# One DVE assignment step per query tile, placed differently in the second head of the first pair

## Chip, cores and metric

The kernel runs on one core of a Trainium2 chip. The metric is the device time of one execution in microseconds, as the median of repeated runs. Engines are named as in the profile: PE is the matrix engine (PEld its weight loads), DVE the vector engine, ACT the scalar engine, POOL GpSimd, SP the engine that only issues DMAs here.

## What is computed

Three stages follow each other: a clustered attention, a mixture of experts that sends each token to one of eight experts, and a gated dense layer. Only the first is touched. Its core:

```python
q_assign = np.argmax(np.einsum('bhsd,hcd->bhsc', q_n, c_n), axis=-1)
k_assign = np.argmax(np.einsum('bhsd,hcd->bhsc', k_n, c_n), axis=-1)
mask = q_assign[:, :, :, None] == k_assign[:, :, None, :]
scores = scale * np.matmul(q, k.transpose(0, 1, 3, 2))
scores = np.where(mask, scores, -1000000000.0)
attn = softmax(scores)          # row maximum, exp, row sum
out = np.matmul(attn, v)
```

There are 2 x 8 = 16 heads of 768 tokens with 64 channels, and 16 cluster centroids for each of the 8 head numbers. Every query and key gets the number of its nearest centroid, and a query sees only keys with the same number.

## The kernel before

Heads are worked through in pairs: pair 0, a hardware loop over the pairs 1 to 6, and pair 7. In a pair, slot 0 is the first head and slot 1 the second. A head has six query tiles of 128 rows, `qt` 0 to 5. Tiles are numbered through as `n = 6 * head + qt`, so the second head of pair 0 has the tiles 6 to 11.

Each engine has an instruction stream of its own, written by hand in program order, and the streams meet only at semaphores. An engine executes its stream in that order. For one query tile `n` they do this:

- PE `head` (L1465): the scores of tile `n` into one of two PSUM buffers (`score_high` L1402 and `score` L1423, two matmuls each); then the six transposes of the probabilities of tile `n - 2` (`transpose_probs`, L1433, in two groups of three, each waiting for DVE to have emptied the previous tile's group, `s_pl`); then, for the head before, a half of the product with v in the tiles with `qt % 3` of 0 and 1 (`probs_v`, L1448 to L1451), or the six small matmuls that turn its result back in the tiles with `qt % 3` of 2 (`turn_back`, L1461).
- DVE `head` (L1100): the row maximum of tile `n` (`neg_max`, L1110); two subtractions that empty the transposed probabilities of tile `n - 2` (`pT_lo`, L1078); in `qt` 0 the row sums of the head before (L1086, L1088); in `qt` 2 and 5 the scaling of its result (`scale_x`, L1097), which waits for `turn_back`.
- ACT `head` (L836): copies of the transposed probabilities of tile `n - 2` (L829), then the exponential of tile `n` (L849); in `qt` 1 and 4 the copy `o_T` (L834) that `turn_back` needs.

Beside this, each pair prepares the assignment masks of the next pair. PE makes the similarities (L1361). DVE finds the assignment in five steps (`assign`, L1051), each of 128x384 elements and each waiting for the one before: step 0 is the maximum (L1055), step 1 compares with it (L1058), step 2 multiplies with the centroid numbers (L1062), step 3 is the minimum (L1065), step 4 writes `one_hot` (L1069) and sends `s_hot`. PE then transposes `one_hot` (`hot_transposes`, L1384, six matmuls), ACT writes the mask rows from that (`make_mask_rows`, L821), and SP sends them by DMA to the operands of the next pair's heads (L471).

In pair 0, PE's `hot_transposes` stands at the end of the third query tile of the second head, behind `turn_back` and ahead of the scores of the fourth tile:

```python
if more and slot == 1 and qt == (2 if first else 1):
    hot_transposes(pp + 1)          # begins with pe.wait_ge(s_hot, pp)
```

ACT's `make_mask_rows` stands in the fourth query tile of that head. DVE runs its steps at the end of a query tile, behind everything else of that tile:

```python
if before and qt % GT == 2:
    scale_x(g - 1, pp - 1 + slot, 1 - slot, qt // GT)
for step in steps.get((slot, qt), ()) if more else ():
    assign(pp + 1, step)
```

`steps` says which steps run in which (slot, query tile). Pair 0 has a table of its own, `first`; there the similarities are ready only in the fifth query tile of its first head, so step 0 runs in (0, 5).

Of the kernel before, what the change touches and what calls it, by code (L numbers as in the profile page):

```python
# [22 lines left out]
def attention_moe_gate(nc, qT, kT, v, cen, w_gate, w1, w2, w_a, w_b, w_out, out):  # L23
# [32 lines left out]
    with ExitStack() as ctx:  # L56
# [316 lines left out]
        def static(j):  # L373
            return isinstance(j, int)
# [637 lines left out]
        def _(dve):  # L1012
# [38 lines left out]
            def assign(pp, step):  # L1051
                s3 = sims.rearrange("p (t c) -> p t c", c=C)
                if step == 0:
                    dve.wait_ge(s_sims, pp + 1)
                    dve.tensor_reduce(sim_max[:, :], s3, AX_X, ALU.max).then_inc(s_smax, 1)  # L1055
                if step == 1:
                    dve.wait_ge(s_smax, pp)
                    dve.tensor_tensor(sim_is_max[:, :, :], s3, sim_max[:, :].unsqueeze(2).to_broadcast([P, 4 * QT, C]),  # L1058
                                      ALU.is_equal).then_inc(s_sism, 1)
                if step == 2:  # L1060
                    dve.wait_ge(s_sism, pp)
                    dve.tensor_tensor(sim_idx[:, :, :], sim_is_max[:, :, :], c_minus_ps, ALU.mult).then_inc(s_sidx, 1)  # L1062
                if step == 3:
                    dve.wait_ge(s_sidx, pp)
                    dve.tensor_reduce(first_idx[:, :], sim_idx[:, :, :], AX_X, ALU.min).then_inc(s_sfst, 1)  # L1065
                if step == 4:
                    dve.wait_ge(s_sfst, pp)
                    dve.wait_ge(s_hotT, pp)
                    dve.tensor_tensor(one_hot[:, 2:, 0:C], c_minus_ps,  # L1069
                                      first_idx[:, :].unsqueeze(2).to_broadcast([P, 4 * QT, C]),  # L1070
                                      ALU.is_equal).then_inc(s_hot, 1)

            def evacuate(n, qt, pT_ps=pT_ps):
                half, j = qt // GT, qt % GT
                for part in range(2):
                    dst = (slice(None), half, slice(part * GT, (part + 1) * GT), slice(j * P, (j + 1) * P))
                    dve.wait_ge(s_ph, 2 * n + part + 1)
                    dve.tensor_tensor(pT_lo[dst], pT_ps[part].rearrange("p (k q) -> p k q", q=P),  # L1078
                                      pT_hi[dst].bitcast(F32), ALU.subtract).then_inc(s_pl, 1)

            def row_norm(g, slot):
                dve.wait_ge(s_exp, QT * (g + 1))
                if not static(g) or g >= 1:
                    dve.wait_ge(s_rinv, g)
                    dve.wait_ge(s_x, 2 * g)
                dve.tensor_reduce(row_eps[:, :], row_sum[:, slot], AX_X, ALU.add).then_inc(s_reps, 1)  # L1086
                dve.wait_ge(s_reps, g + 1)
                dve.reciprocal(row_inv[:, :], row_eps[:, :]).then_inc(s_rinv, 1)  # L1088

            def scale_x(g, stored, slot, half):  # L1090
                dve.wait_ge(s_back, 2 * g + half + 1)
                dve.wait_ge(s_rinv, g + 1)
                if half == 0 and (not static(g) or g >= 2):
                    dve.wait_ge(s_rows[slot], stored * 16)
                    dve.wait_ge(s_logit, g - 1)
                tiles = slice(half * GT, (half + 1) * GT)
                dve.tensor_tensor(x_head[:, slot, tiles, :], x_ps, row_inv[:, tiles].unsqueeze(2).to_broadcast([P, GT, XW]),  # L1097
                                  ALU.mult).then_inc(s_x, 1)

            def head(pp, slot):  # L1100
                g = pp * 2 + slot
                more = not static(pp) or pp + 1 < PAIRS
                before = not static(g) or g >= 1
                first = static(pp) and pp == 0
                steps = {(0, 5): (0,), (1, 0): (1, 2), (1, 1): (3, 4)} if first else {
                    (0, 2): (0,), (0, 3): (1,), (0, 4): (2,), (0, 5): (3,), (1, 0): (4,)}
                for qt in range(QT):
                    n = g * QT + qt
                    dve.wait_ge(s_S, n + 1)
                    dve.tensor_reduce(neg_max[:, qt % 2:qt % 2 + 1], scores[qt % 2][:, 0:S], AX_X, ALU.max,  # L1110
                                      negate=True).then_inc(s_max, 1)
                    if before or qt >= 2:
                        evacuate(n - 2, (qt - 2) % QT)
                    if before and qt == 0:
                        row_norm(g - 1, 1 - slot)
# [4 lines that stand above are left out]
                    if static(pp) and pp == PAIRS - 1:  # L1120
                        early_routing(slot * QT + qt)
# [29 lines left out]
            def early_routing(at):  # L1151
                if at == 0:
                    dve.wait_ge(s_hotr, PAIRS)
                    link(dve.tensor_copy(early_e_minus, e_minus[:, 0, :]))
                if at == 1:
                    dve.wait_ge(s_logit, H)
                    choose(0, 0)
                if at == 3:
                    choose(0, 1)
                if at == 4:  # L1160
                    choose(0, 2)
                    link(dve.tensor_copy(l_max[:, batch[0]], early_max))
                if at == 6:
                    choose(0, 3)
                if at == 7:
                    choose(0, 4)

            def pair(pp):
                head(pp, 0)
                head(pp, 1)  # L1170
# [628 lines left out]
```

## Time and profile before

| | |
|---|---|
| median of 3 runs | 816.57 us (816.55 to 816.61) |
| the profiled execution's own time | 816.57 us |
| its span, first to last instruction | 814.8 us |
| PE busy | 806.8 us, 99% of the span |
| DVE, ACT, POOL busy | 456.0, 361.1, 365.0 us |
| granted TensorE clock | 1.000 |

A row of the timeline gives the start of a group of like instructions, its length, the engine, the line, the operation, output and input tiles with their shapes, and how many there are; behind them, in brackets, idle time before it and what ended it. Instructions of one engine overlap at their ends, so the step from one start to the next is shorter than the length of a row. The steps from start to start are what an engine's program costs.

### The profile page before, as it was taken

The page shows a single profiled execution, that of the slowest core. Times are in us where ns is not written, and L with a number is a line of the kernel's source. Part 1 is how long each engine was busy: PE and PEld are TensorE (multiplying, and loading weights), DVE is VectorE, ACT ScalarE, POOL GpSimd, SP SyncE. Part 2 cuts the span into 40 slices and gives each one's busy share as a digit, 9 for nine tenths or more (in the row PEclk, how much of TensorE's full clock was granted, in tenths as well). Part 3 has the DMA queues.
Part 4 walks back from the last instruction along what each step waited for, and adds up shares of the span by engine and source line. Part 5 has one row for each costly group of instructions (what it writes and reads, how often), then busy time and mean ns, then how long its engine had stood idle before and what let it go on. Part 6 is the DMA issues. An engine that isn't in the chain of part 4 may idle for free.

```text
span 814.8 us, 13171 instructions
## 1 busy us (share of the span) xinstructions
PE 806.8 (99%) x4412; PEld 678.6 (83%) x4413; DVE 456.0 (56%) x716; ACT 361.1 (44%) x741; POOL 365.0 (45%) x306
## 2 busy tenths in 40 slices
PE   8999999999999999999999999999999999999997
PEld 5899999999998688888888888888888888888886
DVE  5987987987997989999867004531212112121211
ACT  7877877877886334343443443111212111121112
POOL 6788988988982454455454634000411002010001
PEclk9999999999999999999999999999999999999999
DMA  7463363363242577788767313300101000010001
GB/s 202 114 185 96 102 185 93 101 184 95 63 117 92 168 233 215 246 255 252 211 210 226 106 38 106 114 0 14 31 9 53 1 14 13 1 52 0 1 1 52
DMA packets 48633, 86.59 MB, mean 106 GB/s; under 512 B 17840, under 2 KB 19888, under 8 KB 48592
## 3 DMA queue, kind: packets, MB, share of 16 engines
q1 hardware_dynamic: 41888, 69.36, 29.4%
q0 software_dynamic: 3824, 11.29, 4.6%
q10 hardware_dynamic: 2880, 5.39, 1.8%
q8 instruction: 25, 0.41, 0.2%
q14 instruction: 16, 0.13, 0.1%
HBM read 73.25 MB, written 11.30 MB: 104 GB/s over the span
## 4 chain that ended last, share of the span: by engine, by line
PE 79%; issue 16%; DVE 2%; POOL 1%; DMA 1%; SPq 0%; POOLq 0%; ACT 0%; DVEq 0%
PE bank L1602 9%; PE bank L1670 9%; PE bank L1433 8%; PE bank L1569 7%; PE bank L1571 7%; PE bank L1570 6%; PE bank L1607 4%; PE bank L1402 4%; PE bank L1674 4%; PE bank L1423 4%; PE bank L1449 4%; PE bank L1451 3%; PE bank L1461 2%; PE bank L1361 2%; PE bank L1614 2%
## 5 line engine op out<-in xcount | busy, mean ns | idle before, releaser
L1325 DVE TENSOR_TENSOR ab_raw<-bank,a_sb 128x512 f32<-128x512 f32 x35 | 24.2, 692 | 187.5 <-PE bank L1571 181.7
L1110 DVE TENSOR_REDUCE neg_max<-bank 128x1 f32<-128x768 f32 x96 | 91.4, 953 | 30.3 <-PE bank L1423 29.4
L398 DVE CAST w_split<-stage 128x1024 fp32r<-128x1024 f32 x68 | 67.0, 985 | 72.7 <-PE bank L1607 53.8
L402 DVE TENSOR_TENSOR w_split<-stage,w_split 128x1024 fp32r<-128x1024 f32 x72 | 102.3, 1425 | 2.3
L1078 DVE TENSOR_TENSOR pT_lo<-bank,pT_hi 128x384 fp32r<-128x384 f32 x192 | 97.5, 549 | 2.7 <-ACT pT_hi L829 2.6
L829 ACT ACTIVATE pT_hi<-bank 128x384 fp32r<-128x384 f32 x192 | 84.3, 491 | 32.0 <-PE bank L1433 30.2
L849 ACT ACTIVATE probs<-bank,neg_max 128x768 f32<-128x768 f32 x96 | 87.1, 907 | 12.0 <-DVE neg_max L1110 12.0
L695 POOL TENSOR_TENSOR hT_lo<-hT_raw,hT_hi 128x512 fp32r<-128x512 f32 x38 | 55.4, 1460 | 82.3 <-ACT hT_raw L903 82.0
L1433 PE MATMUL bank<-ident,probs 128*128 128x128 f32 x576 | 80.0, 274 | 0.9 <-DVE pT_lo L1078 0.9
L963 ACT ACTIVATE a_sb<-bank 128x512 f32<-128x512 f32 x35 | 20.9, 597 | 134.8 <-PE bank L1571 125.9
L1670 PE MATMUL bank<-w_split,hT_hi 128*128 (+1 forms) x304 | 79.4, 403 | 0.0
L1602 PE MATMUL bank<-w_split,xT_hi 128*128 (+1 forms) x304 | 78.5, 400 | 0.0
L1569 PE MATMUL bank<-x2T_a,w_split 128*128 128x512 f32 (+1 forms) x200 | 77.0, 385 | 0.0
L1571 PE MATMUL bank<-x2T_a,w_split 128*128 128x512 f32 (+1 forms) x200 | 76.7, 383 | 0.0
L1570 PE MATMUL bank<-x2T_a,w_split 128*128 128x512 f32 (+1 forms) x200 | 75.9, 379 | 0.0
L1433 PEld LDWEIGHTS bank<-ident,probs 128*128 128x128 f32 x576 | 66.0, 141 | 8.1 <-issue 1.9
L1602 PEld LDWEIGHTS bank<-w_split,xT_hi 128*128 128x128 f32 x304 | 55.8, 188 | 11.8
L1670 PEld LDWEIGHTS bank<-w_split,hT_hi 128*128 128x128 f32 x304 | 54.4, 189 | 10.2
L1449 PE MATMUL bank<-pT_lo,v_split 128*64 128x384 f32 x192 | 61.7, 348 | 0.0
L707 POOL CAST token_i<-x 128x2 int32<-128x2 f32 x12 | 2.5, 208 | 122.9 <-PE bank L1626 65.6
L897 ACT ACTIVATE h_relu<-bank 128x512 f32<-128x512 f32 x38 | 22.7, 598 | 77.8 <-PE bank L1607 77.8
L1451 PE MATMUL bank<-pT_hi,v_split 128*128 128x384 f32 x160 | 53.9, 337 | 0.0
(253 smaller groups left out, 1736.2 us busy)
## 6 DMA issues: line engine op xcount, KB each, us to landing
stage<-w SPq DMA_DIRECT2D x64, 512.0 KB
q_raw<-qT SPq DMA_DIRECT2D x32, 192.0 KB, 3.7
k_raw<-kT SPq DMA_DIRECT2D x32, 192.0 KB, 3.8
sorted_y<-y_sb ACTq DMA_DIRECT2D x19, 257.0 KB, 5.0
q_pair<-qT SPq DMA_DIRECT2D x8, 384.0 KB, 4.6
v_raw<-v_keys SPq DMA_DIRECT2D x16, 192.0 KB, 3.7
stage<-w_a SPq DMA_DIRECT2D x6, 512.0 KB
stage<-w_b SPq DMA_DIRECT2D x6, 512.0 KB
```

The lines of the kernel that those rows point to most:

```text
L402: eng.tensor_tensor(dst[:, 1], stage[:, i % STAGES], dst[:, 0].bitcast(F32), ALU.subtract).then_inc(s_cv, 1)
L829: act.activation(pT_hi[:, half, part * GT:(part + 1) * GT, j * P:(j + 1) * P], pT_ps[part].rearrange("p (k q) -> p k q", q=P), ACT.Copy).t ...
L849: act.activation(probs[:, qt % 2], scores[qt % 2][:, 0:S], ACT.Exp, bias=neg_max[:, qt % 2:qt % 2 + 1], accum_out=row_sum[:, slot, qt, 0:1 ...
L1078: dve.tensor_tensor(pT_lo[dst], pT_ps[part].rearrange("p (k q) -> p k q", q=P), pT_hi[dst].bitcast(F32), ALU.subtract).then_inc(s_pl, 1)
L1110: dve.tensor_reduce(neg_max[:, qt % 2:qt % 2 + 1], scores[qt % 2][:, 0:S], AX_X, ALU.max, negate=True).then_inc(s_max, 1)
L1433: last = pe.transpose(pT_ps[part][:, j * P:(j + 1) * P], probs[:, slot, kt * P:(kt + 1) * P], ident[:, :])
L1449: pe.matmul(oT_ps[0:D], v_split[:, slot, kt, 0], pT_lo[:, half, kt], start=False, stop=False)
L1569: pe.matmul(ps, lh, rh, start=first, stop=False)
L1570: pe.matmul(ps, lh, rl, start=False, stop=False)
L1571: return pe.matmul(ps, ll, rh, start=False, stop=last)
L1602: pe.matmul(h_ps[half], xT_hi[:, par, cols(c)], ring((r % 2) * HELD + c, part)[:, cols(half, 512)], start=(c == 0 and part == 0), stop=False)
L1670: pe.matmul(y_ps, hT_hi[:, cols(k)], ring((r % 2) * HELD + C1 + k // 2, part)[:, cols(k % 2, 512)], start=(k == 0 and part == 0), stop=False)
```

## The change

One line of the DVE program. It concerns pair 0 alone, and there the second head: steps 1 and 2 ran in its first query tile and steps 3 and 4 in the second; now step 1 runs in the first, steps 2 and 3 in the second, and step 4 in the third. Nothing else is changed, neither the steps themselves nor any other engine's program.

```diff
-                steps = {(0, 5): (0,), (1, 0): (1, 2), (1, 1): (3, 4)} if first else {
+                steps = {(0, 5): (0,), (1, 0): (1,), (1, 1): (2, 3), (1, 2): (4,)} if first else {
                     (0, 2): (0,), (0, 3): (1,), (0, 4): (2,), (0, 5): (3,), (1, 0): (4,)}
```

## Rows read from the trace of the kernel before

**Rows 1.** The page: busy time by engine, and the granted clock in 40 slices.
```profile
PE 806.8 (99%) x4412; PEld 678.6 (83%) x4413; DVE 456.0 (56%) x716; ACT 361.1 (44%) x741; POOL 365.0 (45%) x306
PEclk9999999999999999999999999999999999999999
```
**Rows 2.** Waits of PE over the whole span: total us, times, longest.
```profile
PE bank L1349 <- POOL ident_bf L564: 2.0, 1, 2.0
PE bank L1433 <- DVE pT_lo L1078: 0.9, 3, 0.4
```
**Rows 3.** Timeline of DVE in the second head: start us, length us, instruction.
```profile
29.32 0.52 DVE L1058 TENSOR_TENSOR sim_is_max<-bank,sim_max 128x384 f32<-128x384 f32 x1
29.87 0.55 DVE L1062 TENSOR_TENSOR sim_idx<-sim_is_max,bank 128x384 f32<-128x384 f32 x1
30.34 0.95 DVE L1110 TENSOR_REDUCE neg_max<-bank 128x1 f32<-128x768 f32 x1
31.21 1.01 DVE L1078 TENSOR_TENSOR pT_lo<-bank,pT_hi 128x384 fp32r<-128x384 f32 x2
32.14 0.54 DVE L1065 TENSOR_REDUCE first_idx<-sim_idx 128x24 f32<-128x384 f32 x1
32.71 0.56 DVE L1069 TENSOR_TENSOR one_hot<-bank,first_idx 128x384 bf16<-128x384 f32 x1
33.19 0.95 DVE L1110 TENSOR_REDUCE neg_max<-bank 128x1 f32<-128x768 f32 x1
34.05 1.01 DVE L1078 TENSOR_TENSOR pT_lo<-bank,pT_hi 128x384 fp32r<-128x384 f32 x2
34.98 0.37 DVE L1097 TENSOR_TENSOR x_head<-bank,row_inv 128x216 f32<-128x216 f32 x1
35.27 0.95 DVE L1110 TENSOR_REDUCE neg_max<-bank 128x1 f32<-128x768 f32 x1
```
**Rows 4.** Timeline of PE over the first three query tiles of that head.
```profile
28.70 0.52 PE L1423 MATMUL bank<-k_hm,q_lm 80*128 80x512 f32 x2
29.06 0.82 PE L1433 MATMUL bank<-ident,probs 128*128 128x128 f32 x6
29.64 0.42 PE L1449 MATMUL bank<-pT_lo,v_split 128*64 128x384 f32 x1
...
31.11 0.51 PE L1423 MATMUL bank<-k_hm,q_lm 80*128 80x512 f32 x2
31.90 0.92 PE L1433 MATMUL bank<-ident,probs 128*128 128x128 f32 x6 [0.28 <-DVE pT_lo L1078]
32.75 0.89 PE L1461 MATMUL bank<-back_w,o_T 128*128 128x72 f32 x6
33.48 0.50 PE L1384 MATMUL bank<-ident_bf,one_hot 128*128 128x128 bf16 x6
33.78 0.59 PE L1402 MATMUL bank<-k_hl,q_hh 128*128 128x512 f32 x2
34.21 0.51 PE L1423 MATMUL bank<-k_hm,q_lm 80*128 80x512 f32 x2
34.75 0.92 PE L1433 MATMUL bank<-ident,probs 128*128 128x128 f32 x6
35.50 0.41 PE L1448 MATMUL bank<-pT_hi,v_split 128*128 128x384 f32 x1
```
**Rows 5.** Timeline of ACT: the copy that `turn_back` waits for.
```profile
32.22 0.48 ACT L834 ACTIVATE o_T<-bank 128x384 f32<-128x384 f32 x1
```
**Rows 6.** Timeline near the start: a like transpose of `one_hot` that waited for DVE.
```profile
13.06 0.36 DVE L1188 TENSOR_TENSOR one_hot<-bank,first_idx 128x192 bf16<-128x192 f32 x1
13.47 0.23 PEld L1392 LDWEIGHTS bank<-ident_bf,one_hot 128*128 128x128 bf16 x4 [0.27 <-DVE one_hot L1188]
```
**Rows 7.** Timeline of PE in its first 7 us: two groups of one matmul form.
```profile
2.05 4.81 PE L1349 MATMUL bank<-ident_bf 128*128 128x512 bf16 x11 [2.05 <-POOL ident_bf L564]
...
6.87 0.81 PE L1349 MATMUL bank<-ident_bf 128*128 128x512 bf16 x3
```

## The prediction

> **What bounds the kernel now.** I read the page first. PE is busy for 806.8 us, 99% of a span of 814.8 us, no other engine for over 56% [rows 1]. So PE's program in its order is the path, and the other engines count only where PE waits for them. The list of PE's waits comes next: after the start-up wait of 2.0 us the largest entry is 0.9 us in three places, for DVE's `pT_lo` [rows 2]. Nowhere later has PE lost much, and nowhere is there slack in which a delay of PE could vanish. A microsecond put into PE's stream should come out at the end of the kernel.
>
> Then the timeline of the stretch that is edited, about 28 to 36 us. DVE has no pause in it: each row of rows 3 begins before the one ahead of it has ended. PE is mostly back to back, with two places where it is late by DVE. The normal step from the second score pair (L1423) to the transposes (L1433) is 28.70 to 29.06, 0.36 us [rows 4]. At 31.11 to 31.90 it is 0.79 us, 0.43 too long. At 34.21 to 34.75 it is 0.54 us, 0.18 too long, and the transposes themselves then take 34.75 to 35.50, 0.75 us to the next group, where 29.06 to 29.64 shows 0.58 without a wait: another 0.17. So DVE, loaded with two extra steps in each of two tiles, costs PE some tenths here. Behind 35.5 us PE is back to back again.
>
> The third thing to see is where the consumer of step 4 stands. PE's `hot_transposes` (L1384) ran at 33.48, directly behind `turn_back` [rows 4], while `one_hot` was ready at 32.71 + 0.56 = 33.27 [rows 3]. PE did not wait for it, but the margin was only 0.2 us. The change doesn't move that consumer.
>
> **The change part by part.** No instruction is added or taken away. Three things move: step 2 from the first tile into the second, step 4 from the second into the third, and with them the maxima and subtractions between them. I replay DVE from the start of step 1, 29.32, which nothing in the change touches. The steps from start to start are from rows 3: a `neg_max` 0.87 (30.34 to 31.21), a pair of `pT_lo` 0.93 (31.21 to 32.14), an assignment step ahead of other work 0.47 (29.87 to 30.34), a step ahead of the one that needs its result 0.57 (32.14 to 32.71), `scale_x` 0.29 (34.98 to 35.27).
>
> First tile: step 1 is now ahead of `neg_max`, 0.47, so `neg_max` of tile 7 starts at 29.79 instead of 30.34, 0.55 earlier. Second tile: 0.87 and 0.93, so step 2 starts at 31.59; 0.57 to step 3, at 32.16; 0.47 to the `neg_max` of tile 8 at 32.63, where it stood at 33.19. Its scores are there in both cases: their second pair started at 31.11 and is over by 31.11 + 0.51 = 31.62 [rows 4]. Third tile: 0.87 and 0.93 to `scale_x` at 34.43, 0.29 to step 4 at 34.72, which takes 0.56 [rows 3]. `one_hot` is ready at 35.28 instead of 33.27, 2.01 us later, since a maximum, two subtractions and `scale_x` now stand ahead of it.
>
> PE meanwhile gains a little. `pT_lo` of the second tile now starts at 30.66 and its first half (half of 1.01, a little more) is done by 31.2, before PE's scores end; so the transposes start at 31.11 + 0.36 = 31.47 and the 0.43 us is gone. `turn_back` waits for ACT's `o_T`, which moves with the maximum from 32.22 to about 31.67 and ends at 32.15 [rows 5]; `turn_back` starts at about 32.2 instead of 32.75, and is over after its usual step of 33.48 - 32.75 = 0.73, at 32.9 [rows 4]. What is late next is `hot_transposes`: it waits for `one_hot` at 35.28. The nearest case of this same wait is at the start of the kernel: `one_hot` ends at 13.06 + 0.36 = 13.42, PE loads its first piece at 13.47 [rows 6], 0.05 us. The wait of `pT_lo` by the transposes is the other bound: its first half ends at about 31.76 (31.21 + 0.55) and PE starts at 31.90, 0.14. I take 0.05, the same operation on both sides. PE starts `hot_transposes` at 35.33, and stood idle for some 2.2 us. Against 33.48 this is 1.85 us late. The 0.55 us gained before it are swallowed: PE only arrives earlier at the wait.
>
> Queued behind the waiting instruction on PE is everything: the scores of tile 9, the transposes of tile 7 and all that follows. DVE and ACT can't go on either, since the maximum of tile 9 needs those scores. But they finish what they have, and that pays a little back. In the new order the subtractions of tile 6 are done by 34.43 + 0.1 and `scale_x` by 34.8, long before PE asks for them, so the two late steps behind the scores of tile 9, 0.18 and 0.17 us, vanish [rows 4]. PE's net shift behind them is 1.85 - 0.18 - 0.17 = 1.50 us.
>
> Everything later moves with PE: ACT's mask rows come behind the exponential of tile 9, the DMAs of the masks behind them, and the first heads of pair 1 which need them are moved by the same 1.5 us. I count nothing for them, since their cover (the two and a half tiles between) moves whole; if that cover were gone the masks could cost more, which is in the range.
>
> The sum: 816.57 us is the time of the profiled execution, span 814.8 and 1.8 around it, and it equals the median of the runs. 816.57 + 1.50 = 818.07, which I give as 818.1.
>
> The bounds: if the 0.35 us do not come back and the wake takes 0.14, it is 1.94, so 818.5. If the engines, which are fresh after the pause, also spare PE the largest later wait for `pT_lo`, 0.4 us [rows 2], it is 1.10, so 817.7.
>
> **The rivals.** (1) Slower by more: the clock falls. In its first 4.8 us PE ran the matmul of L1349 eleven times in 4.81 us, a spacing of about 0.42, and right behind three of them in 0.81, about 0.22 [rows 7]: the lower of the two levels, 1.2 against 2.4 GHz, after the 2.05 us in which PE had done nothing. Later the clock is at full level in all slices, and PE is never idle for more than 0.4 us in one piece [rows 1, 2], so the trace has no example of a 2.2 us pause in mid-work. If the clock falls, the price by these rows is a stretch like the first, 4.8 us at half speed, 2.4 us lost: 818.1 + 2.4 = 820.5. It decides if the pause drops the level at all. Against it speaks that PE works at once behind and right up to the pause. I give it 0.08.
>
> The Trainium skill (TensorE: Matmul & The Clock Gate, "What's actually happening") says that the array is throttled by default and that only activity releases it; by that rule a long enough pause costs this rival's time, and no row here shows how it answers one in mid-work.
>
> (2) Not slower: the delay is given back where PE joins something that isn't driven by PE. That needs a later wait of PE of at least 1.5 us, on a DMA or on a routing result whose own start isn't moved. The list shows no such wait on the matmuls [rows 2], and PE's 99% leaves only 8 us of non-busy time, of which 2 are at the start. If it did occur, all 1.5 would go: 816.6. Chance 0.06.
>
> (3) Faster: `hot_transposes` doesn't hold PE. Then the gains alone stand: 0.43, 0.18 and 0.17, together 0.78, giving 815.8. It would need `one_hot` to be ready by about 32.9, when PE gets there, but DVE has 5.96 us of work in front of that from 29.32 on (the replay), all of it at durations that the trace shows. Or the engine would have to pass a waiting instruction, and PE's matmuls stand in program order in all rows. Chance 0.02.
>
> The Trainium skill (the same page, "Step-by-step: what each phase is for") says that PE may pull weight loads ahead of running matmuls, but that matmuls stay in order; by the first half alone one would hope for rival 3, by the second the stall stands.
>
> **How the numbers follow.** The forecast as worked out has 0.84. The likeliest time is 818.1. With what a measurement of this kernel can tell apart, about 0.2% or 1.6 us, the line lies at 818.2, just above it. Of the forecast's 0.84 I put 0.52 below the line and 0.32 above, since the center lies 0.1 us under it and the bounds reach from 817.7 to 818.5. Within 0.2%: 0.52 + 0.06 (rival 2) = 0.58. Slower by over 0.2%: 0.32 + 0.08 = 0.40. Faster: 0.02. The range runs from 817.5 to 818.9: the bounds, widened by 0.2 below and 0.4 above, the latter for masks that come late. The rivals, 0.16 together, stay outside.
>
> **What would show it.** In the profile of the changed kernel: `neg_max` of tile 7 0.55 us earlier, at 29.8; the transposes of tile 6 with no wait, at 31.5; step 4 behind `scale_x`, at 34.7; a PE wait of L1384 for DVE `one_hot` L1069 of about 2.2 us, by far the longest after the start; the scores of tile 9 at 35.6; from about 37 us on every PE row 1.5 us later than before, and a span of 816.3. Wrong would be: no such wait of L1384; matmuls behind it at double spacing or a granted clock under full (rival 1); or a shift of 1.5 us at 40 us that has shrunk at 280 us or at the end (rival 2).

## The result, and the profile after

The changed kernel takes 819.47 us in the median of 17 runs (817.81 to 821.05), the kernel before 816.61 us (816.30 to 817.11). The ratio is 1.003, 95% interval 1.0023 to 1.0037: slower by 0.3%. The forecast was 818.1 in a range of 817.5 to 818.9, so the median lies outside.

The median alone hides what happened. The 17 times fall into three groups, and the mean granted TensorE clock of each run goes with them:

| runs | time us | mean clock |
|---|---|---|
| 7 | 817.81 to 818.09 | 0.999 to 1.000 |
| 8 | 819.30 to 819.68 | 0.997 to 0.998 |
| 2 | 820.70 and 821.05 | 0.996 |

All runs of the kernel before are at 0.999 or 1.000. The seven in the first group have the forecast time; eight are some 1.6 us above it and two some 2.7 to 3.0 us. A mean clock of 0.998 over 818 us is what some 3.3 us at half clock leave, one of 0.996 some 6.5 us (an estimate, since the mean is given to three digits): the two groups fit one short and one twice as long stretch at the lower level. The profiled execution is one of the first group: time 818.01 us, span 816.3 us, clock 1.000.

First its waits of PE over the span, which answer [rows 2]:

```profile
PE bank L1384 <- DVE one_hot L1069: 2.2, 1, 2.2
PE bank L1349 <- POOL ident_bf L564: 2.0, 1, 2.0
PE bank L1433 <- DVE pT_lo L1078: 0.6, 2, 0.4
```

The top one is new: PE sat idle for 2.2 us in front of `hot_transposes`. The timeline of DVE in the second head, against [rows 3]:

```profile
29.46 0.52 DVE L1058 TENSOR_TENSOR sim_is_max<-bank,sim_max 128x384 f32<-128x384 f32 x1
29.89 0.95 DVE L1110 TENSOR_REDUCE neg_max<-bank 128x1 f32<-128x768 f32 x1
...
31.69 0.54 DVE L1062 TENSOR_TENSOR sim_idx<-sim_is_max,bank 128x384 f32<-128x384 f32 x1
32.27 0.55 DVE L1065 TENSOR_REDUCE first_idx<-sim_idx 128x24 f32<-128x384 f32 x1
32.73 0.95 DVE L1110 TENSOR_REDUCE neg_max<-bank 128x1 f32<-128x768 f32 x1
33.60 1.01 DVE L1078 TENSOR_TENSOR pT_lo<-bank,pT_hi 128x384 fp32r<-128x384 f32 x2
34.53 0.37 DVE L1097 TENSOR_TENSOR x_head<-bank,row_inv 128x216 f32<-128x216 f32 x1
34.82 0.55 DVE L1069 TENSOR_TENSOR one_hot<-bank,first_idx 128x384 bf16<-128x384 f32 x1
36.73 0.96 DVE L1110 TENSOR_REDUCE neg_max<-bank 128x1 f32<-128x768 f32 x1 [1.36 <-PE bank L1423]
```

Step 4 (L1069) stands behind `scale_x` (L1097). Behind it DVE itself is idle for 1.36 us, since the scores of tile 9 are late. PE over the same stretch, against [rows 4]:

```profile
31.61 0.82 PE L1433 MATMUL bank<-ident,probs 128*128 128x128 f32 x6
32.30 0.89 PE L1461 MATMUL bank<-back_w,o_T 128*128 128x72 f32 x6
35.42 0.51 PE L1384 MATMUL bank<-ident_bf,one_hot 128*128 128x128 bf16 x6 [2.23 <-DVE one_hot L1069]
35.74 0.60 PE L1402 MATMUL bank<-k_hl,q_hh 128*128 128x512 f32 x2
36.17 0.52 PE L1423 MATMUL bank<-k_hm,q_lm 80*128 80x512 f32 x2
36.53 0.82 PE L1433 MATMUL bank<-ident,probs 128*128 128x128 f32 x6
37.10 0.42 PE L1448 MATMUL bank<-pT_hi,v_split 128*128 128x384 f32 x1
...
38.93 0.82 PE L1433 MATMUL bank<-ident,probs 128*128 128x128 f32 x6
```

The wait of 2.23 us is there, the small waits around it are gone (the transposes directly behind the scores at 31.61 and 36.53, the product with v 0.57 us behind them at 37.10). From here on PE keeps its delay: `turn_back` stands at 40.41 in the kernel before and at 41.99 after, later at 252.53 and at 254.04, and the spans differ by 1.5 us at the end. The DMA of the mask rows (L471), first the row of before, then that of after, moves by the same 1.6 us:

```profile
38.16 0.55 SPq L471 DMA_DIRECT2D q_lm<-hot_rows  x1
```
```profile
39.72 0.55 SPq L471 DMA_DIRECT2D q_lm<-hot_rows  x1
```

### The profile page after: what moved, and what is told of

The parts are those of the page before. It is cut to its first block, busy times and chain, and to the rows that moved or that the text cites. A ratio compares the mean times of both kernels' runs of the same rounds, so it can differ in the third digit from the quotient of the medians.

```text
span 816.3 us, 13171 instructions
## 1 busy us (share of the span) xinstructions
PE 806.2 (99%) x4412; PEld 678.8 (83%) x4413; DVE 453.5 (56%) x716; ACT 360.8 (44%) x741; POOL 367.1 (45%) x306
## 4 chain that ended last, share of the span: by engine, by line
PE 79%; issue 16%; DVE 3%; POOL 1%; DMA 0%; POOLq 0%; ACT 0%; DVEq 0%
PE bank L1602 9%; PE bank L1670 9%; PE bank L1433 7%; PE bank L1569 7%; PE bank L1571 7%; PE bank L1570 6%; PE bank L1607 4%; PE bank L1674 4%; PE bank L1402 4%; PE bank L1423 4%; PE bank L1449 4%; PE bank L1451 3%; PE bank L1461 2%; PE bank L1361 2%; PE bank L1614 2%
## 5 line engine op out<-in xcount | busy, mean ns | idle before, releaser
L398 DVE CAST w_split<-stage 128x1024 fp32r<-128x1024 f32 x68 | 65.2, 959 | 75.0 <-PE bank L1607 54.2
```

## The experiments

Each edit is shown against the changed kernel, that of "The pause without the change" against the kernel before. The code is cut to the lines around it.

**The pause filled with work.** If PE's idle 2.2 us make the clock fall in some of the runs, work in their place must stop that without moving anything else.

```diff
                     if more and slot == 1 and qt == (2 if first else 1):
+                        if first:
+                            pe.wait_ge(s_exp, n)
+                            for _ in range(9):
+                                pe.matmul(scores[1][:, 0:512].rearrange("p (a q) -> p a q", q=P), ident_bf[:, :],
+                                          ident_bf[:, :].unsqueeze(1).to_broadcast([P, 4, P]), start=True, stop=True)
                         hot_transposes(pp + 1)
```

> The changed kernel, and ahead of hot_transposes in the third tile nine plain bf16 matmuls of 512 columns into the free score buffer: at the spacing of 0.22 us that the spins of L1349 have at the full clock they fill 1.9 of the 2.2 us in which PE waited for one_hot. They start nothing earlier and delay nothing. Theory A (the clock falls in part of the executions because PE is idle for 2.2 us): every execution at a mean clock of 1.000, all times between 817.6 and 818.4, median 818.0. Theory B (the spread of 817.8 to 821.05 has another source, such as DMAs or POOL work that the moved schedule meets): the wait for DVE ends when it did, the spread stays, median near 819.5 and clocks of 0.996 to 0.998 in about half of the runs.

Measured: median 818.01 us, 817.66 to 818.30 in 11 runs, all at a clock of 0.999 or 1.000. The timeline of PE in this kernel:

```profile
32.49 0.89 PE L1461 MATMUL bank<-back_w,o_T 128*128 128x72 f32 x6
33.22 2.11 PE L1492 MATMUL bank<-ident_bf 128*128 128x512 bf16 x9
35.61 0.51 PE L1384 MATMUL bank<-ident_bf,one_hot 128*128 128x128 bf16 x6 [0.29 <-DVE one_hot L1069]
```

`hot_transposes` starts no earlier (3.12 us behind the start of `turn_back`, as in the changed kernel), so the delay of 1.5 us is the same, and it is paid in every run. What is gone is everything above 818.3. Work that serves nothing makes the median 1.5 us faster (1.2 if the kernel before, at 816.39 beside these runs and at 816.61 beside those of the changed kernel, is taken as the measure). Theory A holds, B falls: the wait for DVE ends where it did, yet no execution is slow. The fillers do two things at once, though: they shorten the idle piece and they add work, and these runs can't say which of the two counts.

**The pause made longer.** DVE repeats one multiplication four times ahead of step 4.

```diff
+                    if first and (slot, qt) == (1, 2):
+                        dve.wait_ge(s_sfst, 1)
+                        for _ in range(4):
+                            link(dve.tensor_tensor(sim_idx[:, :, :], sim_is_max[:, :, :], c_minus_ps, ALU.mult))
                     for step in steps.get((slot, qt), ()) if more else ():
```

> The changed kernel with four repeats of step 2's multiplication, each waiting for the one before, ahead of step 4: by the chained spacing of 0.58 us they make one_hot 2.3 us later, and PE's idle piece 4.5 us. Without any effect on the clock the time is 818.0 + 2.3 = 820.3. Theory A: the clock falls in nearly every execution, so the profiled one too, a mean clock of 0.998 or less, and 1.6 us or more on top: 822 or above; the trace shows matmuls at double spacing behind the pause. Theory B: 820.3 in the fastest and the same spread of up to 3 us above, clock not tied to it.

Measured: median 821.82 us, 821.54 to 822.22, all four runs at a clock of 0.996 or 0.997. Four of four fell. The median is a little under the 822 of theory A. The profiled execution has a span of 820.2 us. Its busy time by stretches; behind the start and end stand the length, the busy time of PE, PEld, DVE, ACT and POOL with their instructions, the granted clock (1.00 is full), the DMA share and GB/s:

```profile
30.00:33.00 3.00, 3.00 (x22) 2.73 (x21) 2.97 (x6) 2.74 (x7) 2.83 (x3) 1.00 0.08 29
33.20:34.60 1.40, 0.00 (x0) 0.00 (x0) 1.40 (x4) 0.92 (x2) 1.32 (x2) 1.00 0.02 6
34.70:37.70 3.00, 0.00 (x0) 0.00 (x0) 2.84 (x6) 0.00 (x0) 1.26 (x2) 0.50 0.00 0
37.70:41.40 3.70, 3.66 (x18) 3.38 (x19) 1.21 (x2) 0.63 (x2) 0.00 (x0) 0.50 0.00 0
41.50:45.00 3.50, 3.50 (x24) 3.20 (x23) 2.55 (x5) 3.48 (x7) 0.00 (x0) 1.00 0.08 15
```

The clock is already at its lower level (0.50, which is 1.2 of 2.4 GHz) in the last 3 us of the idle piece, and stays there for 3.7 us of work behind it. The expected time without a fall was 820.3, so by the times the fall costs 1.5 us. The rows give 1.75: from the start of `hot_transposes` to the transposes of tile 8 it is 37.74 to 43.00 here, 5.26 us, and 35.42 to 38.93, 3.51 us, in the changed kernel's profiled execution, which did not fall.

```profile
37.74 0.82 PE L1388 MATMUL bank<-ident_bf,one_hot 128*128 128x128 bf16 x6 [4.58 <-DVE one_hot L1069]
43.00 0.82 PE L1437 MATMUL bank<-ident,probs 128*128 128x128 f32 x6
```

Either figure is near half of 3.7 us: the low part that lies in the idle piece costs nothing.

**The pause shortened in part.** The first experiment's edit with five and with two filling matmuls.

> As the run with nine filling matmuls, but five: 1.1 us filled, PE idle for about 1.1 us of the 2.2 in one piece. With no fall of the clock the time is 818.0 in every run. Theory A1 (the chance of a fall grows with the length of the idle piece, and 2.2 us lies where it is about one half): none or one in ten executions at a clock of 0.998 and 819.5. Theory A2 (any idle piece of a microsecond or more is enough, by luck of the moment): about half of the executions as with the changed kernel.

> Two filling matmuls, some 0.5 us filled, PE idle for about 1.7 us in one piece. Theory A1: a share of falls clearly under that of the changed kernel (10 of 17), 1 to 4 of about eleven; the others at 818.0, those at 819.6. Theory A2: half. Median 818.0 to 818.2 by A1, 819.5 by A2.

Measured with five: median 817.97 us, 817.65 to 818.51, 11 runs, none under 0.999. With two: median 819.31 us, 817.77 to 819.86, 9 runs, of which five at 0.998 (819.31 to 819.86) and four at 1.000 (817.77 to 818.48). The waits of PE in the one and in the other:

```profile
PE bank L1384 <- DVE one_hot L1069: 1.2, 1, 1.2
```
```profile
PE bank L1384 <- DVE one_hot L1069: 1.8, 1, 1.8
```

Each theory is right once. With five fillers it came out as A1 says, none of 11 runs fell; with two as A2 says, about half of them (5 of 9, against 10 of 17 in the changed kernel) and a median of 819.3, where A1 had clearly fewer than half and 818.0 to 818.2. So the length of the piece matters, but between 1.2 and 1.8 us the chance rises from nothing seen to about a half, and from there to 2.2 us these two kernels show no further rise. The profiled execution with two fillers fell, and shows what the usual fall costs. Its timeline of PE:

```profile
35.65 0.51 PE L1384 MATMUL bank<-ident_bf,one_hot 128*128 128x128 bf16 x6 [1.80 <-DVE one_hot L1069]
35.97 0.60 PE L1402 MATMUL bank<-k_hl,q_hh 128*128 128x512 f32 x2
36.40 0.52 PE L1423 MATMUL bank<-k_hm,q_lm 80*128 80x512 f32 x2
36.76 1.02 PE L1433 MATMUL bank<-ident,probs 128*128 128x128 f32 x6
37.43 0.67 PE L1448 MATMUL bank<-pT_hi,v_split 128*128 128x384 f32 x1
...
38.53 0.52 PE L1451 MATMUL bank<-pT_hi,v_split 128*128 128x384 f32 x1
38.85 0.52 PE L1449 MATMUL bank<-pT_lo,v_split 128*64 128x384 f32 x1
...
40.73 0.82 PE L1433 MATMUL bank<-ident,probs 128*128 128x128 f32 x6
```

and its stretches:

```profile
33.00:35.60 2.60, 0.85 (x6) 0.35 (x5) 2.60 (x6) 1.28 (x3) 2.44 (x3) 1.00 0.01 3
35.60:37.20 1.60, 1.55 (x15) 1.47 (x16) 0.24 (x1) 0.00 (x0) 0.84 (x1) 1.00 0.00 0
37.30:40.60 3.30, 3.30 (x13) 2.82 (x12) 1.59 (x3) 2.73 (x5) 0.00 (x0) 0.50 0.02 5
40.70:44.00 3.30, 3.30 (x27) 3.12 (x25) 2.53 (x4) 2.39 (x6) 0.00 (x0) 1.00 0.58 173
```

From the transposes of tile 7 to those of tile 8 it is 36.76 to 40.73, 3.97 us. In the changed kernel's profiled execution, which did not fall, the same way is 36.53 to 38.93, 2.40 us. The fall costs 1.57 us, which is what parts the groups of 818.0 and 819.5. The clock is at its upper level through the whole pause and for 1.6 us of work behind it, and falls only then, with PE fully busy. The profiled executions of the next two experiments fell as well, and in the same way: they are at 1.00 until 1.5 and 1.7 us behind the start of `hot_transposes` and at 0.50 in the 3.3 us that follow.

The page of this fallen execution, which averages over slices of 20 us, doesn't show the fall:

```profile
PEclk9999999999999999999999999999999999999999
```

**The pause a little longer.** The second experiment's edit with one repeat.

> The changed kernel with one repeat of step 2's multiplication ahead of step 4: one_hot 0.6 us later, PE idle for 2.8 us in one piece, 818.6 without a fall. Theory A1: a fall in three quarters of the executions or more, median 820.2 or above (1.6 us for the shorter fall seen with the changed kernel, up to 3 for the longer). Theory A2: half of them, values at 818.6 and 820.2 in equal parts.

Measured: median 820.12 us, 819.08 to 821.64, 5 runs: 0.998 twice (820.10, 820.12), 0.996 twice (821.49, 821.64), and 0.999 once (819.08). PE's wait for `one_hot` is 2.8 us. Four of five fell, which fits A1, though four of five can't be told from a half. The fifth has a clock that the kernel before shows too, and is 0.4 us above the 818.6 without a fall.

**The pause without the change.** The kernel before, its steps where they were, with four linked repeats ahead of step 4.

```diff
                     for step in steps.get((slot, qt), ()) if more else ():
+                        if first and step == 4:
+                            dve.wait_ge(s_sfst, 1)
+                            for _ in range(4):
+                                link(dve.tensor_tensor(sim_idx[:, :, :], sim_is_max[:, :, :], c_minus_ps, ALU.mult))
                         assign(pp + 1, step)
```

> The kernel before, its steps in their old places, with four linked repeats of step 2's multiplication ahead of step 4 in the second tile. DVE and PE are both held up by 4 x 0.58 = 2.3 us; PE waits at hot_transposes for about 2.2 us, as in the changed kernel, though nothing is moved. Without a fall: 816.4 + 2.3 = 818.7. If the idle piece alone makes the clock fall, about half of the executions are at a clock of 0.998 and 1.6 us above, 820.3. If it is something of the changed order instead, all are at 818.7 and a clock of 1.000.

Measured: median 820.68 us, 819.68 to 821.43, 5 runs at clocks of 0.998, 0.998, 0.997, 0.996 and 0.996. Its wait of PE (L1388 is the line of `hot_transposes` here):

```profile
PE bank L1388 <- DVE one_hot L1069: 2.0, 1, 2.0
```

A pause in the same place with the old order makes the clock fall too. It fell in five of five, more often than I expected from its length; with five runs I can't say that this differs from ten of 17. The fall needs the idle piece and not the changed order of DVE's steps.

**The consumer moved as well.** The changed DVE order, with `hot_transposes` in the fourth tile behind the transposes of the probabilities.

```diff
+                    if first and (slot, qt) == (1, 3):
+                        hot_transposes(pp + 1)
                     if more and slot == 0 and qt in sim_tiles:
...
-                    if more and slot == 1 and qt == (2 if first else 1):
+                    if more and slot == 1 and qt == 1 and not first:
```

> The changed DVE order, and PE's hot_transposes of pair 0 moved from the end of the third tile to the fourth, right behind its transposes of the probabilities. The consumer then comes about 2 us behind step 4's old place. If the cost of the change is the wait of PE for one_hot alone, it is gone, PE is idle nowhere, the clock stays at 1.000 in every run, and what is left is the early gain as far as DVE lets it through: the transposes of tile 7 wait for DVE's pT_lo of tile 6, which is at 34.1 either way, so of the 0.78 us I expect 0.4: 816.2. If moving steps has a price of its own (DVE order, later masks), it is 816.6 or more.

Measured: median 816.41 us, 816.25 to 817.05, 11 runs at 0.999 or 1.000, against 816.39 for the kernel before, measured beside it: ratio 1.0001, 0.9992 to 1.0010. No cost of the change is left that could be told from nothing, so the price was the wait and not the moved steps. The gain that I expected can't be seen; the interval, 0.7 to 0.8 us to either side, would still hold one of 0.2 to 0.4. PE's timeline shows where it went:

```profile
33.34 0.52 PE L1423 MATMUL bank<-k_hm,q_lm 80*128 80x512 f32 x2
34.21 0.92 PE L1433 MATMUL bank<-ident,probs 128*128 128x128 f32 x6 [0.35 <-DVE pT_lo L1078]
35.34 0.51 PE L1384 MATMUL bank<-ident_bf,one_hot 128*128 128x128 bf16 x6 [0.20 <-DVE one_hot L1069]
35.66 0.42 PE L1448 MATMUL bank<-pT_hi,v_split 128*128 128x384 f32 x1
```

PE comes to the transposes earlier and waits there for DVE, and, against my expectation that it is idle nowhere, a second time for `one_hot`. The product with v begins at 35.66, where it began at 35.50 [rows 4].

**Half of the change.** Step 1 in the first tile, steps 2 to 4 all in the second.

```diff
-                steps = {(0, 5): (0,), (1, 0): (1,), (1, 1): (2, 3), (1, 2): (4,)} if first else {
+                steps = {(0, 5): (0,), (1, 0): (1,), (1, 1): (2, 3, 4)} if first else {
```

> Step 1 in the first tile as in the changed kernel, but steps 2, 3 and 4 all in the second, so that step 4 keeps its old place ahead of the third tile's maximum. This is the half of the change that lightens the first tile, without the late step 4. one_hot is then ready at about 33.3, hot_transposes waits at most 0.4 us, and the clock stays at 1.000. DVE does the same work before the maximum of tile 8 as before, so the gain of 0.43 us at the transposes of tile 6 is given back there: 816.5, not to be told from 816.6. If the lighter first tile is worth its 0.55 us, 816.1.

Measured: median 816.36 us, 816.18 to 816.78, 11 runs at 0.999 or 1.000, ratio 1.0000 (0.9991 to 1.0009). As expected: a lighter first tile alone shows no gain. The transposes of tile 6 come at once, and PE then waits 0.28 us for `one_hot` and 0.15 for `pT_lo`, together the 0.43 us that it had gained:

```profile
33.35 0.51 PE L1384 MATMUL bank<-ident_bf,one_hot 128*128 128x128 bf16 x6 [0.28 <-DVE one_hot L1069]
34.77 0.92 PE L1433 MATMUL bank<-ident,probs 128*128 128x128 f32 x6 [0.15 <-DVE pT_lo L1078]
```

None of the variants beats the kernel before.

## Why the prediction was wrong, point by point

- **DVE replayed.** Right. `neg_max` of tile 7 at 29.89 (29.79 worked out), of tile 8 at 32.73 (32.63), `scale_x` at 34.53 (34.43), step 4 at 34.82 (34.72). This execution is 0.14 us later from before the stretch on (step 1 at 29.46 for 29.32), which the replay could not contain. One reading was too strong: not each row of [rows 3] begins before the one ahead of it has ended. Two steps that need the result of the one ahead begin 0.03 us behind its end, at 29.87 and 32.71. The sum goes by starts and is untouched.
- **The wait of `hot_transposes`.** Right: 2.23 us for 2.2, at 35.42 for 35.33. (From its own 32.9, the start of `turn_back` and its step, the prediction would get 2.4; the last of those matmuls ends later than the step says, at 33.19, and the idle time counts from there.) The wake: `one_hot` ends at 34.82 + 0.55 = 35.37, PE starts 0.05 later, the lower of the two bounds.
- **What the pause gives back.** Right: both small waits are gone, net shift 1.6 us at 40 us and 1.5 at 252 us and in the spans. The span is 816.3 as forecast, and the executions without a fall have 817.8 to 818.1 for 818.1.
- **Masks, and slack later on (rival 2).** Right to count nothing: the DMAs of the mask rows move with PE (38.16 to 39.72), and no delay is given back.
- **Rival 1, the clock.** Here it failed, twice. The mechanism was named, but its chance was put at 0.08, and it happened in 10 of 17 runs, so the median itself lies in that case. The step that failed is the reason given against it, "that PE works at once behind and right up to the pause": the trace of before has no idle piece of PE over 0.4 us after the start, so it had no row on which a chance that low could rest. In its place the runs show that work right up to the pause and at once behind it protects from nothing: in three profiled executions the clock fell 1.5 us or more after PE had gone back to work. Nor does a row of nines in PEclk [rows 1] mean a full clock throughout, as the prediction read it; the page of a fallen execution has the same row. And the price was mis-sized: 2.4 us, from the 4.8 us of slow matmuls at the start, where the usual fall measures 1.57 us. Added to a correct 818.0 this is 819.6, where eight runs lie; the two at 820.7 and 821.05 are 2.7 and 3.0 above, and by their mean clock of 0.996 were at the lower level for about twice as long. No trace of such an execution of the changed kernel was kept.
- **The range.** It left the clock outside, with a chance of 0.08, among rivals of 0.16 together. With a chance that the rows could not settle, it should have reached to 820.5.

The faster rival was rightly given next to nothing. The line of 0.2% was a hair's breadth above the forecast time, and the fall of the clock moved the median over it.

## What to carry to other kernels

When an instruction is moved later on one engine, ask first where its consumer stands on the engine that sets the end; moved without its consumer, the step turned a margin of 0.2 us into a wait of 2.2 us, and moved together with it no loss could be measured. Price a new pause of TensorE twice: its length less what it gives back, and a fall of the clock, which here added 1.6 us in eight of 17 runs and 2.7 to 3.0 in two; look at all the runs with their clocks, since one profiled execution can be of the kind without it. Where such a pause can't be avoided, filling matmuls in it can be worth having: with five or nine of them the median was 818.0 instead of 819.5 us, though the pause itself is still paid.

## What the runs showed of the hardware

An idle piece of TensorE in the middle of dense work was followed by a clock of 1.2 GHz in some executions and not in others, of the same kernel (the length is that in the one profiled execution of each):

| idle in one piece, us | kernel | runs with a lower mean clock |
|---|---|---|
| 0.3 | nine fillers | 0 of 11 |
| 1.2 | five fillers | 0 of 11 |
| 1.8 | two fillers | 5 of 9 |
| 2.0 | before, with a pause | 5 of 5 |
| 2.2 | the change | 10 of 17 |
| 2.8 | one repeat | 4 of 5 |
| 4.6 | four repeats | 4 of 4 |

I had not expected that 1.8 us could be enough, nor that the fall can come 1.6 us after the pause, when TensorE is busy again, so that the slow stretch is all work and costs in full. In the kernel with 4.6 us the slow stretch began within the pause, and of a longer time at the low level only 1.5 to 1.75 us was lost.

The granted clock of the profile leaves out the start of the kernel. In the kernel before it reads 1.00 for a stretch in which the spacing of the matmuls shows the lower level (about 0.42 us where the same form right behind takes 0.22 [rows 7]), so a mean clock of 1.000 here speaks of what comes after:

```profile
2.00:6.50 4.50, 4.45 (x11) 1.49 (x11) 1.62 (x12) 2.55 (x6) 3.30 (x15) 1.00 0.89 275
```
 The Trainium skill (TensorE: Matmul & The Clock Gate, "What's actually happening") says that the clock's default is throttled and that activity releases it. These runs agree: the clock fell behind idle pieces, and it was back at its upper level while PE worked (with two fillers 0.50 up to 40.60, 1.00 from 40.70). The same section remarks, of the start of a kernel, that the change of level doesn't come at a fixed point of the program; that the same kernel falls in one execution and not in the next looks like the same thing in mid-kernel, which no run here proves. What the work around the pause has to do with the chance was not tried: all of these pauses lie at the same place, between `turn_back` and `hot_transposes`.
